# Inverse row sums turned through HBM, x taken out of PSUM unscaled and multiplied two tiles later

## The reference, cut to what matters

```python
scores = np.where(keep, scale * q @ k.T + bias, -1e9)
a = np.exp(scores - max)                 # per head, 768 x 768, only the band is not zero
a = a / (np.sum(a, axis=-1, keepdims=True) + 1e-09)
x = a @ v                                # 2 batches, 8 heads, 768 rows, 64 columns
gate = sigmoid(causal_conv(x, conv_w)); x = (gate * (x @ w_val)) @ w_out
h = relu(x @ w_in); out = (h * sigmoid(conv(h))) @ w_out2
```

## Time and profile before

| | |
|---|---|
| median of 3 runs | 273.87 us (273.57 to 274.32) |
| profiled execution, its own time | 274.46 us |
| its span, first to last instruction | 271.8 us |
| granted TensorE clock, mean | 0.998 |
| PE busy | 266.6 us, 98% |
| DVE busy | 185.9 us, 68% |
| ACT busy | 158.8 us, 58% |
| POOL busy | 35.8 us, 13% |
| attention loop, start of `qk(2)` to start of `val(0)` | 38.88 to 100.62 us |

### The profile page before, as it was taken

How to read it: one execution, slowest core, us unless ns; L and a number is a source line. 1 busy time by engine, 2 the same in 40 slices (tenths; PEclk the granted TensorE clock), 3 DMA queues, 4 the chain that set the end, 5 groups by cost and what they waited for, 6 DMA issues and landing times.

```text
span 271.8 us, 4494 instructions
## 1 busy us (share of the span) xinstructions
PE 266.6 (98%) x1574; PEld 211.1 (78%) x1574; DVE 185.9 (68%) x457; ACT 158.8 (58%) x362; POOL 35.8 (13%) x63
## 2 busy tenths in 40 slices
PE   8999999999999999999999999999999999999995
PEld 7544478888788888888888888888888888888883
DVE  0488388878899992698970796997508998992000
ACT  1051588889999991655542607865628748753110
POOL 1011017777133220000000000000000000000000
PEclk9999999999999999999999999999999999999999
DMA  6999825646662000000000000000000002104021
GB/s 203 361 376 311 300 60 181 181 129 167 188 190 77 4 0 2 5 2 0 0 0 0 2 0 0 1 2 0 0 0 2 0 0 99 59 0 154 0 93 62
DMA packets 12152, 21.83 MB, mean 80 GB/s; under 512 B 1760, under 2 KB 2272, under 8 KB 12000
## 3 DMA queue, kind: packets, MB, share of 16 engines
q1 hardware_dynamic: 10976, 20.52, 23.2%
q10 hardware_dynamic: 1152, 1.01, 1.1%
HBM read 18.37 MB, written 3.15 MB: 79 GB/s over the span
## 4 chain that ended last, share of the span: by engine, by line
PE 92%; ACT 5%; DVE 1%; issue 1%
PE ps L535 20%; PE ps L536 20%; PE ps L537 20%; PE ps L419 9%; PE ps L506 7%; PE ps L466 6%; PE ps L484 6%; ACT prob L676 3%; PE ps L492 2%; PE ps L434 1%; PE ps L430 1%; ACT probT L689 1%; DVE prob L934 1%; ACT invT L683 0%; ACT g L715 0%
## 5 line engine op out<-in xcount | busy, mean ns | idle before, releaser
L676 ACT ACTIVATE prob<-prob,low 128x256 f32<-128x256 f32 (+1 forms) x96 | 46.0, 485 | 4.3 <-DVE low L934 4.3
L959 DVE SCALAR_TENSOR_TENSOR g<-xT,cw,g 128x512 f32<-128x512 f32 x48 | 32.8, 748 | 2.2 <-ACT g L715 2.2
L790 ACT ACTIVATE h<-ps 128x512 f32<-128x512 f32 x24 | 14.0, 595 | 31.3 <-PE ps L537 31.3
L934 DVE CUSTOM_DVE_ANT_0 prob<-ps,bias 128x256 f32<-128x256 f32 x80 | 30.0, 413 | 2.6 <-PE ps L466 2.6
L535 PE MATMUL ps<-hghA,w2h 128*128 128x512 f32 x64 | 24.9, 390 | 0.0
L537 PE MATMUL ps<-gh,Wl 128*128 128x512 f32 x64 | 24.9, 390 | 0.0
L537 PE MATMUL ps<-hghA,w2l 128*128 128x512 f32 x64 | 24.9, 390 | 0.0
L535 PE MATMUL ps<-gh,Wh 128*128 128x512 f32 x64 | 24.9, 389 | 0.0
L536 PE MATMUL ps<-gl,Wh 128*128 128x512 f32 x64 | 24.9, 389 | 0.0
L536 PE MATMUL ps<-hglA,w2h 128*128 128x512 f32 x64 | 24.9, 389 | 0.0
L419 PE MATMUL ps<-win,w1t 128*128 128x512 f32 x56 | 24.6, 596 | 0.0
(11 more groups left out here) (100 smaller groups left out, 544.8 us busy)
## 6 DMA issues: line engine op xcount, KB each, us to landing
q_rows<-in_q SPq DMA_DIRECT2D x12, 256.0 KB, 4.6
kW<-in_k SPq DMA_DIRECT2D x12, 256.0 KB, 4.4
v_own<-in_v SPq DMA_DIRECT2D x12, 256.0 KB, 2.9
out<-xT SPq DMA_DIRECT2D x5, 512.0 KB, 2.8
w<-in_w SPq DMA_DIRECT2D x8, 256.0 KB, 11.9
v_win<-in_v SPq DMA_DIRECT2D x10, 192.0 KB, 3.0
prob<-in_wval SPq DMA_DIRECT2D x1, 1024.0 KB, 9.8
win<-in_win SPq DMA_DIRECT2D x1, 1024.0 KB, 12.0
```

Source lines behind the costliest of these rows:

```text
L676: act.activation(part, part, ACT.Exp, scale=-1.0, bias=low[:, t % 2, i:i + 1], accum_out=total[:, t % 2, i:i + 1]).then_inc(exp_done, 1)
L790: act.activation(h_cols(m, c), pieces(HB(m), c), ACT.Relu).then_inc(relu_done, 1)
L934: dve.tensor_tensor_reduce(prob[:, t % 2, i, cols], SC(f, e)[:, i % HH // 2, cols], table, -SCALE, 3.0e38, ALU.add, ALU.min, low[:, t % 2, ...
L959: dve.scalar_tensor_tensor(out=pieces(g[:, m, :], c), in0=x_cols(m, c, tap - PAD1), scalar=cw1[:, m, tap:tap + 1], in1=pieces(g[:, m, :], ...
```

## The change

The inverse sums no longer pass GpSimd, TensorE and ScalarE. VectorE turns the 8 inverses of each row in 32 by 32 squares (128 x 32 elements, `turn_inverse` on the vector queue). SyncE writes the result to HBM as rows per head, waits for that write, and reads it back spread over partitions with two DMAs of 64 partitions. There are two slots of `invT`; the last two tiles use a slot of the key ring instead. ScalarE copies `PO` to `xT` unscaled (`take_x(t - 1)`, in iteration t behind its second copy of turned exponentials), `pv(t)` waits for that copy, and VectorE multiplies the tile in place at the start of iteration t + 2. The high parts of x for chunk 0 move from ScalarE to GpSimd, which also clears the edges of h; the first taps start one tile later; one early convolution step moves behind the loop; `val(1)` and the work around it no longer wait for all of x.

```diff
-TAPS_FROM = N // P
-EARLY_STEPS = {t: 1 if t < TILES - 3 else 2 for t in range(TAPS_FROM + 1, TILES - 1)}
+TAPS_FROM = N // P + 1
+EARLY_STEPS = {t: 1 + t % 2 for t in range(TAPS_FROM + 1, TILES - 1)}
+LATE_INVERSES = TILES - 2
+SQUARE = 32
...
+        inv_turned = nc.dram_tensor("inv_turned", (TILES, SQUARE, P), f32, kind="Internal").ap()
...
+            def turn_inverse(t):
+                slot = t % 2
+                sp.wait_ge(inverse_done, t + 1)
+                sp.dma_start(inv_turned[t].rearrange("h (b q) -> b h q", q=SQUARE), inv_rows[:, slot, :]).then_inc(inv_sent[slot], 16)
+                sp.wait_ge(inv_sent[slot], 16 * (t // 2 + 1))
+                if t >= 2:
+                    sp.wait_ge(x_ready, t - 1)
+                for e in range(2):
+                    sp.dma_start(invT_of(t)[e * D:(e + 1) * D, :, :], inv_turned[t, e:H:2, :].partition_broadcast(D)).then_inc(invT_in[slot], 16)
...
-                for t in range(RING, TILES):
-                    load_q(t)
-                    load_k(t)
-                    load_v(t)
+                for t in range(TILES):
+                    if t + RING < TILES:
+                        load_q(t + RING)
+                        load_k(t + RING)
+                    turn_inverse(t)
+                    if t + RING < TILES:
+                        load_v(t + RING)
...
                 if t >= 1:
-                    pe.wait_ge(x_ready, t)
+                    pe.wait_ge(x_raw, t)
...
                     for j in range(PAIRS):
                         turn(t, j)
-                    spread_inverse(t)
                     pv(t)
...
+            def take_x(t):
+                act.wait_ge(pv_done, t + 1)
+                act.activation(xT[:, :, t // TPB, x_at(t):x_at(t) + P], PO, ACT.Copy).then_inc(x_raw, 1)
...
                     copy_t0(t, 2)
+                    if t >= 1:
+                        take_x(t - 1)
                     exp_of(t + 1, 2)
                     exp_of(t + 1, 3)
-                    copy_inverse(t)
...
+            def turn_inverse(t):
+                dve.wait_ge(reciprocal_done, t + 1)
+                if t >= 2:
+                    dve.wait_ge(inv_sent[t % 2], 16 * (t // 2))
+                dve.transpose(inv_rows[:, t % 2, :], inv[:, :]).then_inc(inverse_done, 1)
 
             def scale_x(t):
-                dve.wait_ge(pv_done, t + 1)
-                dve.wait_ge(invT_copied, t + 1)
-                dve.tensor_tensor(xT[:, :, t // TPB, x_at(t):x_at(t) + P], PO, invT[:, :, :], ALU.mult).then_inc(x_ready, 1)
+                dve.wait_ge(x_raw, t + 1)
+                dve.wait_ge(invT_in[t % 2], 32 * (t // 2 + 1))
+                tile = xT[:, :, t // TPB, x_at(t):x_at(t) + P]
+                dve.tensor_tensor(tile, tile, invT_of(t), ALU.mult).then_inc(x_ready, 1)
...
+                dve.memset(inv[:, :], 0.0).then_inc(inv_zero, 1)
+                dve.wait_ge(inv_zero, 1)
...
                 for t in range(TILES - 1):
-                    if t >= 1:
-                        scale_x(t - 1)
+                    if t >= 2:
+                        scale_x(t - 2)
                     score(t + 1, 0)
                     score(t + 1, 1)
                     inverse(t)
                     score(t + 1, 2)
+                    turn_inverse(t)
                     score(t + 1, 3)
```

More of the change, by code:

```diff
@@ L92, in program @@
         sb("below_inv", [P, 2, N], where=over_g)
-        inv_wide = sb("inv_wide", [P, H, D], where=over_g)
-        invT = sb("invT", [P, PAIRS, P], where=over_g)
+        invT = sb("invT", [P, 2, PAIRS, P], where=over_g)
         over_g.close()
@@ L246, in k_windows, with copied, invT_of @@
             return 2 * (t + 1) - 1 - (t >= TPB)
+        def copied(t, j):
+            return (t0_copied, t1_copied)[j % 2], 2 * t + j // 2 + 1
+        def invT_of(t):
+            return kW[:, 0, t % 2, :, :] if t >= LATE_INVERSES else invT[:, t % 2, :, :]
         def first_of_batch(t):
@@ L411, in _ @@
                 for k in range(CT):
-                    split_x(0, k)
+                    split_x(k)
+            pool.wait_ge(x_ready, TILES)
+            for edge in (0, HROW, 2 * HROW):
+                pool.memset(h[:, :, edge:edge + 1], 0.0).then_inc(h_edges, 1)
         @block.tensor
@@ L486, in turn @@
                 last.then_inc(tr_done, 1)
[L488 to L493, removed]
             def pv(t):
@@ L596, in _ @@
                 val(0)
+                pe.wait_ge(x_ready, TILES)
             def hid(c):
@@ L979, in conv1, with split_x_low, first_gate @@
                 conv1_pair(c, 1, range(1, K1))
+            def split_x_low(c, k):
+                dve.wait_ge(xh_done, CT * c + k + 1)
+                dve.tensor_tensor(pieces(xl[:, k, :], c), x_cols(k, c), pieces(xh[:, k, :], c).bitcast(f32), ALU.subtract).then_inc(xl_later, 1)
+            def first_gate(taps):
+                for tap in taps:
+                    conv1_pair(0, 1, (tap,))
+                    split_x_low(1, tap - 1)
             MASKS = 8
@@ L1080, in _ @@
                         next_step += 1
-                assert next_step == 2 * (K1 - 1)
-                scale_x(TILES - 2)
+                scale_x(TILES - 3)
                 inverse(TILES - 1)
+                turn_inverse(TILES - 1)
                 copy_t1(TILES - 1, 1)
                 copy_t1(TILES - 1, 3)
+                for step in range(next_step, 2 * (K1 - 1)):
+                    early_conv1(step)
+                scale_x(TILES - 2)
+                first_gate((1, 2, 3))
                 scale_x(TILES - 1)
+                first_gate((4,))
             with dve.Else():
@@ L1129, in low2 @@
                 dve.tensor_tensor(hgl[c][:, two, :], hg[c][:, two, :], hgh[c][:, two, :].bitcast(f32), ALU.subtract).then_inc(hl_done, 1)
-            dve.wait_ge(x_ready, TILES)
-            for edge in (0, HROW, 2 * HROW):
-                dve.memset(h[:, :, edge:edge + 1], 0.0).then_inc(h_edges, 1)
-            def split_x_low(c, k):
-                dve.wait_ge(xh_done, CT * c + k + 1)
-                dve.tensor_tensor(pieces(xl[:, k, :], c), x_cols(k, c), pieces(xh[:, k, :], c).bitcast(f32), ALU.subtract).then_inc(xl_later, 1)
-            for tap in range(1, K1):
-                conv1_pair(0, 1, (tap,))
-                split_x_low(1, tap - 1)
             for m in range(CT):
```

86 lines of the change are left out of this document (37 added, 49 removed).

## The result

The changed kernel takes 282.92 us (median of 4 runs, 281.15 to 284.31) against 274.10 before (273.57 to 274.47): ratio 1.0314, interval 1.0278 to 1.0351, **8.8 us slower**. Forecast were 278.7, with a range of 275.4 to 283.8. The profiled execution is the fastest of the four (281.15), so its trace explains 7.6 us, 279.4 of span against 271.8, and not the whole 8.8.

The account below looks back on a forecast made before the run. TensorE, busy 98% of the span, was taken to bound the kernel. ScalarE's wait +2.4 and SyncE's late inverses +2.4 made +4.8 us, 273.87 to 278.7 us; range for 8 in 10: 275.4 to 283.8.

Parts of the forecast that it names:

- iteration 0, `qk(1)` to `qk(2)`: First loop iteration, without `take_x`: spread no longer delays `qk(2)`, VectorE's new memset and transpose cost 0.3; -0.35 us.
- full iterations, each: Iterations 1 to 4 and 8 to 10: `pv` waits for `take_x` behind ScalarE's second copy, 6.72 us, 0.37 longer.
- iterations 5 to 7, ScalarE's wait only: Iterations with short tile 6 and first taps, by walking ScalarE's list: 17.96 us for 17.29, +0.7.
- last tile: Two `val` parts stand in front of its `pv`, so it waits for nothing and gains 0.53 us.
- first term: Attention loop: TensorE's `pv` held by ScalarE's `take_x`, less the removed spread, summed over all iterations; +2.4 us.
- queue, lateness: SyncE's rounds of 7.4 us fall behind; inverses of tiles 5 to 7 late by 1.2, 1.7, 2.4; +2.4 us.
- clock behind a gap: TensorE's granted clock might fall in the loop through its new idle time; given little, in no sum.
- W: Time for the write of turned inverses to land while SyncE waits: taken as 3.7 us, between 2.0 and 4.8.
- the prediction's own slope: Seven SyncE rounds: each 0.1 us of the write's landing time costs 0.7 us from 3.35 on.
- TensorE's gaps: Rival: 0.9 us idle per iteration lowers the clock, up to 5.8 us per tile; 0.07 together with a much slower queue.
- second term: SyncE's queue falls behind and inverses reach VectorE late: +2.4 us, not added up over tiles.
- The rule beside the rows: Skill's fixed 2.0 us plus bytes per DMA: write lands in 2.04, no queue loss, 276.3 us.

Follow-up runs that it names:

- experiment 1: The changed kernel with SyncE's wait for the write and its two reads moved behind the v loads: 276.63 us, ratio 1.0048 to the kernel before.
- experiment 2: The changed kernel with `take_x(t - 1)` moved to the start of iteration t, SyncE's queue as changed: 282.34 us, ratio 1.0285 to the kernel before.
- experiment 8: The changed kernel with the write to HBM done and waited for twice: 298.37 us in one run.
- 7: The changed kernel with `take_x` early and write, wait and reads issued by GpSimd: 286.99 us profiled, 285.01 to 291.11 over four runs.
- experiment 5: The kernel of experiment 1 with three chained spare products on VectorE ahead of iteration 8's first score: 279.50 us, ratio 1.0188 to the kernel before.
- 6: The kernel of experiment 1 with six chained spare products on VectorE ahead of iteration 8's first score: 284.64 us, ratio 1.0375 to the kernel before.
- experiment 3: The changed kernel with the edits of experiment 1 and experiment 2 together: 271.25 us, ratio 0.9878 to the kernel before.
- experiment 9: The kernel of experiment 3 with GpSimd's first split of x waiting for VectorE's first convolution step: 272.28 us, ratio 0.9928 to the kernel before.
- experiment 10: The kernel of experiment 3 with SyncE writing the turned inverses ahead of the q and k loads: 271.58 us, ratio 0.9887 to the kernel before.
- experiment 12: The kernel of experiment 3 with three convolution steps in the loop where there were seven: 270.88 us, ratio 0.9885 to the kernel before.
- Experiment 4: The changed kernel with the third turn of iteration 7 issued five times, to fill TensorE's gap: 282.84 us, ratio 1.0293 to the kernel before.

## Why the prediction was right in sign and short in size

By the spans it is +7.6 where +4.8 was forecast. The measured terms are 2.2 (the first), 0.3 (a later start of the loop in the profiled execution, which is chance), 2.3 (the queue) and 2.8 (the clock):

| step of the prediction | forecast | measured |
|---|---|---|
| iteration 0, `qk(1)` to `qk(2)` | -0.35 | 0.0 (5.17 and, in experiment 1, 5.18, for 5.14) |
| full iterations, each | +0.37 | +0.32 |
| iterations 5 to 7, ScalarE's wait only | +0.7 | +0.5 (experiment 1) |
| last tile | -0.53 | -0.5 |
| first term | +2.4 | +2.2 (experiment 1) |
| queue, lateness | +2.4 | +2.3 |
| clock behind a gap | little, in no sum | +2.8 |

*ScalarE's wait.* Right, and taken from the right rows: the full iteration is 6.68 for 6.72, and experiment 2 takes the wait away and gets 5.82 for 5.83. The gap of 0.79 in each iteration does not touch the clock: it is 1.00 from 38 to 72 us.

*Iteration 0.* Mis-sized by 0.4. The removed spread gave nothing, because VectorE's last copy ends later than forecast: at 38.75 (38.33 + 0.42), 4.75 behind the start of `qk(1)` where it was 4.09, so 0.66 later and not 0.3. (The copy that ends at 38.08 is the one before, of turn 1.) Behind it stand the 4 products and the 0.4 us that I had counted. The transpose costs 0.13 and the list ahead of the scaling, with the memset, 0.17 more, about as estimated; what I had left out is the 128 x 8 scaling ahead of the reciprocal, which takes 0.57 for 0.17, beside a cast on GpSimd, which no longer waits for the inverses there and works ahead. `qk(1)` itself starts at 34.00 in the changed kernel, 33.74 before and 33.68 in experiment 1, whose lists are the same up to there as the changed kernel's; that 0.3 differs from one execution to the next.

*SyncE's queue.* The mechanism is shown by experiments 1 (wait hidden, gone) and 8 (doubled); in 7 the lag moved with the wait. Its total was right by a path that was not, which is luck. W came out at 3.3 to 4.4 for 3.7 (at 4.4 the prediction's own slope gives 283.6, not the 283.8 of its range). The two reads take 0.6 each to issue for the 0.47 that I took from the loads (whose five take 2.21 by the earlier trace rows, not 2.25), and single rounds were longer, 8.59 for the one before tile 5, in which a k load took 1.14 to issue. So tile 5's inverses landed at 80.2 for 78.6 and were late by 2.3 for 1.2 (limit 77.00 + 0.9). Against experiment 1, which has the same lists without the lateness, iteration 7 less the slow `pv` is 10.60 - 1.71 - 6.85 = 2.04 longer, and iteration 6, where VectorE waited 2.30 for tile 4's inverses, 0.22 (5.38 for 5.16): the forecast had tile 4's just in time. Tiles 6 and 7 were not late at all, since iterations 7 and 8 had become 5.0 us longer and gave SyncE the time. The lateness is not added up, as the prediction says, but I had not let TensorE's own slowing count as time for the queue.

*The step that failed.* It is the rival "TensorE's gaps": "No row before shows a fall, and I give it little." I asked whether the regular 0.9 us gap would lower the clock, and it does not. I did not ask it of the gap that my own second term makes: a late tile stops TensorE for over 2 us at one place. There the clock falls and 2.8 us are lost on top. Experiments 5 and 6 show it alone, in a kernel that is otherwise at 2.4 GHz. The order of causes matters: mend the queue and the fall mostly goes with it, the clock being 0.999 to 1.000 in all ten runs of experiment 1 and all four of experiment 3. Not always, though: 9, 10 and 12 are built on experiment 3, and five of their 20 runs have clocks of 0.992 to 0.994. Nor does every long gap bring a fall: in experiment 2 TensorE idled 2.77 us and went on at 2.4 GHz (rows in the last section). So the price of 2.8 us is what a fall cost here; what decides whether one comes stays open.

*What else stays open.* The median lies 1.8 us above the profiled execution. The other three runs have spans of 280.7 to 282.5 at clocks of 0.988 to 0.994. Experiment 4 shows that the fall can strike another iteration, but what their extra 1.3 to 3.1 us consist of was not profiled.

*The rule beside the rows.* The first write's 2.0 us, out of an empty queue, agrees with the fixed 2.0 us of the Trainium skill (DMA: Bandwidth & Descriptors, Anatomy of one DMA — SWDGE (gpsimd) path), and so does experiment 8's second write. The Trainium skill gives it for DMAs that GpSimd issues, and these are SyncE's. Behind loads it is short by 1.3 to 2.4, and the trace decides. The 256 KB store that the prediction set beside it agrees with the fixed part alone: with the bytes the Trainium skill's formula makes 2.6 us, an estimate, and the row has 2.0. Of the Trainium skill's rule, on the same page, that few outermost rows confine a DMA to few engines (Rules for kernel authors) nothing shows in the time: with 4 outermost the write takes what a 256 KB store takes. How many engines it ran on, no run here shows.

## What to carry to other kernels

A DMA whose landing is awaited by the issuing queue holds up all that stands behind it there, in every round: add up everything that the queue issues in a period, with the wait, and compare with the period of the work it feeds; if loads can be issued between the write and its wait, put them there. Where a forecast makes TensorE wait at one place for more than its usual pause, work out the time with the lower clock behind it as well, and keep both: it came in experiments 4, 5 and 6 and failed to come behind the longest gap of experiment 2. And when two waits are removed, look for the one that sets the period: removing the other alone gave 0.6 us here, within the noise, behind the first it gave 5.4.

## What the runs showed of the hardware

**TensorE's clock can fall behind short single gaps, and need not behind longer ones.** Idle 1.33 and 0.79 us with 0.63 of work between (experiment 5) was followed by a granted clock of 0.56 over the next 3.2 us; idle 1.62 and 0.26 (experiment 10) by 0.53 over 74.8 to 78.4. In experiment 8 idle 1.47 and 0.79 with 0.63 between was not followed by a fall, 1.00 from 67.7 to 73.0, and in the next iteration 1.67 and 0.68, again with 0.63 between, was: 0.50 over 77.0 to 79.9. Gaps of 1.34 in experiment 3 and of 0.79 and 0.70 in experiment 12 had none behind them, and neither had the longest of experiment 2, from TensorE's timeline:

```profile
99.04 0.63 PE L502 MATMUL ps<-ident,prob 128*128 128x128 f32 x4 [2.77 <-ACT probT L693]
...
101.49 2.00 PE L489 MATMUL ps<-kW,q_rows 64*128 64x256 f32 x16
```

The granted clock is 1.00 from 99.0 to 103.4, and `pv` takes its 1.89. The length of a gap alone does not decide.

**VectorE and GpSimd hold each other up.** In the changed kernel two convolution steps beside GpSimd's split took 2.42 us where two take 1.41; the split's product beside a convolution step took 1.59 for 1.27. In experiment 9 a scaling of 128 x 8 elements took as long as the GpSimd product beside it, and 0.26 two tiles earlier. VectorE's timeline of that kernel, and then GpSimd's:

```profile
71.95 0.26 DVE L960 TENSOR_SCALAR total_eps<-total 128x8 f32<-128x8 f32 x1
...
84.86 1.25 DVE L960 TENSOR_SCALAR total_eps<-total 128x8 f32<-128x8 f32 x1
```

```profile
84.81 1.27 POOL L405 TENSOR_TENSOR xl<-xT,xh 128x512 fp32r<-128x512 f32 x1
```

The Trainium skill says that a GpSimd instruction and a VectorE instruction in a two-port mode, or with two inputs in SBUF where GpSimd reads SBUF too, take a shared pair of ports by an exclusive lock, held for a whole instruction (SBUF — State Buffer, SBUF: two separate sides); the trace agrees, 1.25 beside 1.27.
